# Attention and two feed-forwards on one core: another order of the last eight attention units, and an earlier load of the program's flag on VectorE

## The reference

```
scores = q @ k.T / 8 + alibi bias;  keep = key < 8 (global) or 0 <= query - key < 96 (local)
attention = softmax(where(keep, scores, -1e9)) @ v               # 8 heads of 64
h = x @ w_in;  g = (a0 + a1 h + a2 h^2 + a3 h^3) / (1 + |b0||h| + |b1| h^2 + 1e-6);  x = g @ w_out   # 512 -> 2048 -> 512
h = x @ w2_in; solu = h * softmax(h); out = layernorm(solu) * g_ln @ w2_out                           # 512 -> 1024 -> 512
```

## Time and profile before

| | us |
|---|---|
| median of 3 runs | 481.54 (480.85 to 481.79) |
| the profiled execution's own time | 480.79 |
| its span in the profile | 478.90 |
| TensorE busy in the span | 467.9 |
| VectorE busy in the span | 376.2 |
| ScalarE busy in the span | 270.0 |
| granted clock of TensorE, mean | 1.00 of full speed |

### The profile page before, as it was taken

The page is one execution under the profiler, slowest core; times in us unless marked ns, Lnnn a source line. Parts: engine busy times, 40 slices in busy tenths (PEclk is TensorE's granted clock), DMA queues, the critical chain, the costliest instruction groups (busy, mean ns, idle before and its releaser), DMA issues.

```text
span 478.9 us, 7527 instructions
## 1 busy us (share of the span) xinstructions
PE 467.9 (98%) x2734; PEld 382.6 (80%) x2734; DVE 376.2 (79%) x685; ACT 270.0 (56%) x477; POOL 60.4 (13%) x135
## 2 busy tenths in 40 slices
PE   7999989999999999999999999999999999999997
PEld 5667778888888878888887888888888888888885
DVE  6899989999999989778889999999685555555550
ACT  6999998656565555555556445443553333333341
POOL 5989850000000000000000000000000000000000
PEclk9999999999999999999999999999999999999999
DMA  8989864000000000000033445331012222222201
GB/s 294 365 323 335 297 239 179 1 0 1 0 1 0 1 1 0 1 1 1 5 105 89 139 138 170 104 88 44 10 35 67 66 66 66 74 67 76 68 23 44
DMA packets 25665, 42.91 MB, mean 90 GB/s; under 512 B 2080, under 2 KB 16800, under 8 KB 24480
## 3 DMA queue, kind: packets, MB, share of 16 engines
q1 hardware_dynamic: 23760, 36.64, 22.5%
q0 software_dynamic: 1296, 5.24, 3.6%
q10 hardware_dynamic: 576, 0.60, 0.4%
HBM read 33.04 MB, written 3.15 MB: 76 GB/s over the span
## 4 chain that ended last, share of the span: by engine, by line
PE 85%; ACT 8%; DVE 4%; issue 1%; DMA 0%; DVEq 0%; ACTq 0%
PE ps L1220 9%; PE ps L1221 9%; PE ps L1222 9%; PE ps L1152 8%; PE ps L1153 8%; PE ps L1154 8%; ACT probs L499 6%; PE ps L1285 5%; PE ps L1283 5%; PE ps L1284 5%; PE ps L1240 5%; PE ps L1239 5%; PE ps L1238 5%; PE ps L1266 2%; PE ps L1119 1%
## 5 line engine op out<-in xcount | busy, mean ns | idle before, releaser
L1220 PE MATMUL ps<-gate_hi,bank_b_hi 128*128 128x512 f32 x192 | 74.9, 390 | 0.5 <-DVE tok_lo L966 0.5
L1152 PE MATMUL ps<-tok_hi,bank_a_hi 128*128 128x512 f32 x192 | 75.0, 391 | 0.0
L1153 PE MATMUL ps<-tok_lo,bank_a_hi 128*128 128x512 f32 x192 | 74.7, 389 | 0.0
L1222 PE MATMUL ps<-gate_hi,bank_b_lo 128*128 128x512 f32 x192 | 74.7, 389 | 0.0
L1154 PE MATMUL ps<-tok_hi,bank_a_lo 128*128 128x512 f32 x192 | 74.7, 389 | 0.0
L1221 PE MATMUL ps<-gate_lo,bank_b_hi 128*128 128x512 f32 x192 | 74.7, 389 | 0.0
L562 ACT ACTIVATE quad<-ps 128x1024 f32<-128x1024 f32 x23 | 23.7, 1030 | 57.8 <-DVE rest L904 57.8
L499 ACT ACTIVATE probs<-negs,small 128x256 f32<-128x256 f32 (+1 forms) x96 | 45.9, 484 | 1.4 <-DVE small L743 1.1
L459 POOL TENSOR_SCALAR probs<-probs,small 128x256 f32<-128x256 f32 (+1 forms) x96 | 42.6, 467 | 10.7 <-DVE small L754 10.5
L886 DVE SCALAR_TENSOR_TENSOR quad<-quad,small,absh 128x1024 f32<-128x1024 f32 x23 | 29.5, 1282 | 17.9 <-ACT absh L565 17.8
L1220 PEld LDWEIGHTS ps<-gate_hi,bank_b_hi 128*128 128x128 f32 x192 | 36.0, 188 | 8.7 <-issue 1.2
(11 more groups left out here) (107 smaller groups left out, 945.5 us busy)
## 6 DMA issues: line engine op xcount, KB each, us to landing
v_sb<-in_v_win SPq DMA_DIRECT2D x8, 704.0 KB, 6.1
bank_a_raw<-in_w_in SPq DMA_DIRECT2D x4, 1024.0 KB, 8.7
bank_b_raw<-in_w_out SPq DMA_DIRECT2D x4, 1024.0 KB, 7.7
stage_hi<-tok_hi SPq DMA_DIRECT2D x12, 256.0 KB, 2.7
stage_lo<-tok_lo SPq DMA_DIRECT2D x12, 256.0 KB, 2.8
out_dram<-out_sb SPq DMA_DIRECT2D x12, 256.0 KB, 2.0
q_sb<-in_q_t SPq DMA_DIRECT2D x14, 192.0 KB, 4.8
k_sb<-in_k_win SPq DMA_DIRECT2D x7, 384.0 KB, 7.2
```

Of the source, the lines that this page charges most:

```text
L1152: pe.matmul(banks(bank, 1), bank_a_hi[:, f, ws], x_hi, start=(k == 0), stop=False)
L1153: pe.matmul(banks(bank, 1), bank_a_hi[:, f, ws], x_lo, start=False, stop=False)
L1220: pe.matmul(banks(4 + k, 1), bank_b_hi[:, f, ws], g_hi, start=first, stop=False)
L1222: mm = pe.matmul(banks(4 + k, 1), bank_b_lo[:, f, ws], g_hi, start=False, stop=last)
```

## The change

It has two parts.

1. **The tail.** ScalarE and VectorE leave their loops over pairs early and follow a written order, `attend_last`. TensorE takes the values of 40 to 43 at once after the transposition of 42 and 43, then `up(0)`, transposes 44 and 45, `up(1)`, transposes 46 and 47, takes the values of 44 to 47, then `up(2)`. `absh[1]` takes the place of `absh[0]` in the first group, since `absh[0]` lies over a buffer of probabilities. `TAIL` is 42. ScalarE's high parts there are of j = 2, 3, 4 and then 5, VectorE's low parts of tiles 4 to 6, 7 to 9, and 10 and 11.
2. **The head.** VectorE loads the flag before it waits for its two biases; the branch stays behind the two `attend_shift` of unit 0. The two `attend_shift` of unit 1 each wait for their own bias of the window and no longer both for the second.

```diff
 ScalarE
-            for n in range(0, HEADS, 2):
+            for n in range(0, TAIL - 2, 2):
                 attend_pair(n)
-            attend_out(HEADS - 4)
-            gate_first_inputs(0)
-            attend_out(HEADS - 1)
-            split_out_high(0)
-            gate_first_inputs(1)
+            attend_last()
+        def attend_last():
+            attend_copy(TAIL - 2)
+            for h in range(2):
+                attend_exp(HEADS - 2, h)
+            attend_out(TAIL - 4)
+            attend_copy(TAIL)
+            attend_out(TAIL - 1)
+            for h in range(2):
+                attend_exp(HEADS - 1, h)
+            for j in range(POOL_IN // 2, LATE_IN // 2 - 1):
+                split_in_high(j)
+            attend_copy(HEADS - 4)
+            gate_first_inputs(0)
+            split_in_high(LATE_IN // 2 - 1)
+            attend_copy(HEADS - 2)
+            attend_out(HEADS - 4)
+            gate_first_inputs(1)
+            attend_out(HEADS - 1)
+            split_out_high(0)
 VectorE
+        def attend_last():
+            attend_copy(TAIL)
+            attend_low(TAIL - 4)
+            attend_low(TAIL - 1)
+            attend_sums(HEADS - 2)
+            attend_reciprocals(HEADS - 2)
+            for f in range(POOL_IN, IDLE_IN - 2):
+                split_in_low(f)
+            attend_copy(HEADS - 4)
+            for f in range(IDLE_IN - 2, IDLE_IN + 1):
+                split_in_low(f)
+            attend_copy(HEADS - 2)
+            dve.wait_ge(coefs_loaded, 16)
+            dve.wait_ge(act_const, 1)
+            gate_first_poly(0)
+            attend_low(HEADS - 4)
+            attend_low(HEADS - 1)
+            gate_first_poly(1)
+            split_out_low(0)
+            for f in range(IDLE_IN + 1, LATE_IN):
+                split_in_low(f)
-            if h == 0 and n == 1:
-                dve.wait_ge(window_ready, 2)
+            if n == 1:
+                dve.wait_ge(window_ready, h + 1)
...
+        take = windowed(dve)
         dve.wait_ge(bias_ready, 2)
         for h in range(2):
             attend_shift(0, h)
-        take = windowed(dve)
...
-            for n in range(0, HEADS, 2):
+            for n in range(0, TAIL, 2):
                 attend_pair(n)
 TensorE
+            if n >= TAIL:
+                return
-            for n in range(0, HEADS, 2):
+            for n in range(0, TAIL + 2, 2):
                 attend_two(n)
-                if n == HEADS - 4:
-                    pe.wait_ge(shifted_ready, 2 * HEADS)
-                    up(0)
-            for n in (HEADS - 2, HEADS - 1):
+            for n in range(TAIL - 2, TAIL + 2):
                 attend_values(n)
             pe.wait_ge(shifted_ready, 2 * HEADS)
+            up(0)
+            attend_two(HEADS - 4)
             up(1)
+            attend_two(HEADS - 2)
+            for n in range(HEADS - 4, HEADS):
+                attend_values(n)
             up(2)
```

More of the change, by code:

```diff
@@ L250, in attention_feed_forwards @@
     LAG = 4
+    TAIL = HEADS - BLOCKS
     GROUPS = FT // 2
@@ L255, in attention_feed_forwards @@
     LATE_IN = FT - 4
-    IDLE_IN, END_IN = POOL_IN + 5, LATE_IN - 1
+    IDLE_IN = POOL_IN + 5
     def outs_at(n):
-        return [m for m in range(2, DONE_B0 - 1, 3) if n == m + (3 if m % 2 else 4)] + \
-            [m for m in (DONE_B0 - 1,) if n == HEADS - 4]
+        return [m for m in range(2, DONE_B0 - 3, 3) if n == m + (3 if m % 2 else 4)]
     HIGH_ON_DVE = (5, 14, 23, 32)
@@ L535, in attend_pair @@
                     attend_out(m)
-            if k < HEADS:
-                for h in range(2):
-                    attend_exp(k, h)
+            for h in range(2):
+                attend_exp(k, h)
             attend_copy(n)
-            if n == HEADS - 4:
[L541 to L545, removed]
+            for h in range(2):
+                attend_exp(k + 1, h)
+        def attend_last():
+            attend_copy(TAIL - 2)
+            for h in range(2):
+                attend_exp(HEADS - 2, h)
+            attend_out(TAIL - 4)
+            attend_copy(TAIL)
+            attend_out(TAIL - 1)
+            for h in range(2):
+                attend_exp(HEADS - 1, h)
[9 more added lines that the diff above has]
+            split_out_high(0)
         def gate_first_inputs(f):
@@ L551, in gate_first_inputs @@
             act.activation(quad[:, cs], src, ACT.Square).then_inc(first_in, 1)
-            act.activation(absh[0][:, cs], src, ACT.Abs, scale=coef_b[:, 0:1]).then_inc(first_in, 1)
+            act.activation(absh[1][:, cs], src, ACT.Abs, scale=coef_b[:, 0:1]).then_inc(first_in, 1)
             act.activation(poly[:, cs], src, ACT.Identity, scale=coef_a[:, 3:4],
@@ L793, in attend_pair @@
             pr, m = divmod(k, NPB)
[L794 to L801, removed]
-            attend_copy(n)
[L803 to L820, removed]
+            if pr and m == 0:
+                dve.wait_ge(pool_bias, 4 * pr - 2)
@@ new lines, in attend_pair @@
+            attend_shift(k, 0)
+            attend_shift(k, 1)
+            attend_copy(n)
+            attend_sums(n + SUMS_AHEAD)
+            if pr and m == 0:
+                dve.wait_ge(pool_bias, 4 * pr)
+            attend_shift(k + 1, 0)
+            attend_reciprocals(n + SUMS_AHEAD)
+            attend_shift(k + 1, 1)
+            for m_out in outs_at(n):
+                if m_out in HIGH_ON_DVE:
+                    attend_high(m_out)
+                attend_low(m_out)
+        def attend_last():
[19 more added lines that the diff above has]
+                split_in_low(f)
@@ L872, in gate_first_poly @@
             dve.wait_ge(first_in, 3 * f + 2)
-            dve.scalar_tensor_tensor(quad[:, cs], quad[:, cs], abs_b1, absh[0][:, cs], ALU.mult,
+            dve.scalar_tensor_tensor(quad[:, cs], quad[:, cs], abs_b1, absh[1][:, cs], ALU.mult,
                                      ALU.add).then_inc(quad_ready, 1)
```

## The result

The changed kernel is slower: 482.06 us (median of 16 runs, 481.79 to 483.48) against 480.99 for the kernel before, measured beside it (16 runs, 480.56 to 482.15). The ratio is 1.0024, with a 95% interval of 1.0015 to 1.0033, that is +1.15 us (+0.7 to +1.6). The profiled execution took 481.79 us, with a span of 480.0 against 478.9.

The account below looks back on a forecast made before the run. The kernel's end was taken to hang on VectorE's start of group 0's quotient, not TensorE's wait in attention. Tail +1.06 and head -0.18 gave +0.88 us, 482.4 from 481.54; range +0.48 to +1.44, 482.0 to 483.0.

Parts of the forecast that it names:

- slower: Whole-kernel outcome: slower than the kernel before by over 0.2%, 0.96 us; chance 0.38.
- within: Whole-kernel outcome: difference from the kernel before inside 0.2%, 0.96 us; chance 0.52.
- low 47: VectorE's low part of unit 47 in the tail: starts at 77.85 after waiting 0.23 for ScalarE's attend_out(47).
- quotient: VectorE's quotient of group 0, on whose start the kernel's end hangs: moves from 81.63 to 82.69, +1.06 us.
- gain of the head: Kernel start: the earlier flag load on VectorE gains 0.18 us; bounds 0.35 gained to 0.18 lost.
- TensorE's gain stands: Rival: the 0.67 us freed at the transposition of 42 carries to the end, -0.85 in all, 480.7; chance 0.14.
- terms of the tail: Steps on VectorE from the copy of 46 and 47 to group 0's quotient, making it +1.06 us later.
- 0.35 to win: Kernel start: the most gained if unit 1 needn't wait for VectorE's load, starting at 6.57 instead of 6.92.
- cover: VectorE's idle time just before group 0's quotient in the kernel before, waiting for ScalarE's exponential: 0.50 us.
- Nothing moves: Rival: head gives 0.35, VectorE does part of tiles 10 and 11 in time, quotient +0.5, about 481.7; chance 0.10.
- S: Start of VectorE's quotient of group 0: 81.63 before, forecast 82.69, +1.06 us.
- Later still: Rival: quotient later still, kernel measurably slower; a head giving nothing leaves +1.06, 482.6; decides from +0.96 on; chance 0.06.

Follow-up runs that it names:

- e3: Changed kernel with one extra VectorE subtraction of a 512-column tile between tile 11 and the first quotient; ratio to before 1.0042.
- e4: Kernel before with one extra VectorE subtraction of a 512-column tile between tile 11 and the first quotient; ratio to before 1.0002.
- e5: Changed kernel with VectorE's low parts of tiles 10 to 15 one group later, 10 and 11 behind group 0; ratio to before 0.9999.
- e2: Changed kernel with the head's change undone, so the tail alone; ratio to before 1.0041.
- e1: Kernel before with the head's change alone; ratio to before 1.0002.
- e10: Changed kernel, TensorE transposing 44 to 47 and taking their values between up(0) and up(1), other engines reordered, tiles 12 to 15 one group later; ratio to before 0.9976.
- e7: Kernel before with one move: ScalarE copies the pair 40, 41 before the exponentials of 46; ratio to before 0.9999.
- e9: Changed kernel with VectorE's tiles 10 and 11 behind group 2, 12 and 13 behind group 3, 14 and 15 behind group 4; ratio to before 0.9990.
- e6: Changed kernel with gate_first_poly(1) in front of the low part of unit 47 on VectorE; ratio to before 1.0013.

## Why the prediction was right

The forecast was +0.88 us within 0.48 to 1.44. Measured was +0.24%, +1.15 us, inside the range; the interval, +0.7 to +1.6, reaches a little beyond it. The trace gives +1.07 at `up(8)`. The mechanism was the one forecast, and the size was 0.2 us short. The measured value is just over the 0.2% that I had set as the bound of no change, so it falls into the case "slower", to which I had given 0.38, and not into the likeliest, "within", with 0.52; the interval holds the bound. The absolute forecast of 482.4 stood on a median of three runs, 481.54; the kernel before had 480.99 over 16 runs, and so the changed kernel came to 482.06 although the loss was larger than forecast.

| step | predicted, without the head's gain | measured, with it |
|---|---|---|
| transposition of 42 | 64.28 | 64.24 |
| up(0), held by low 41 | 67.19 | 67.26 |
| transposition of 46 | 73.74 | 73.74 |
| VectorE's copy of 46 | 74.51 | 74.50, after 1.10 of waiting |
| attend_out(44), attend_out(47) | 75.15, 77.25 | 75.15, 77.25 |
| low 47 | 77.85, waits 0.23 | 77.86, waits 0.16 |
| quotient | 82.69, +1.06 | 82.71, +1.08 |
| up(8) | +1.06 | 105.16, +1.07 |
| gain of the head | 0.18 | 0.07 at unit 1, 0.10 at unit 40 |

- **That the end hangs on the quotient** is shown by e3 and e4 (0.60 against 0.02 for the same tile) and by e5, where taking two tiles off the chain brings quotient and `up(8)` back. The rival that TensorE's gain stands is refuted with it. The waits of TensorE at `down(0)`, `up(6)` and `up(8)`, 1.17 against 0.12, are the same loss seen on the other engine.
- **The terms of the tail** added up to 1.06. The near match of the positions in the table flatters the forecast: with the head's 0.18 in it the quotient should have come at 82.5. Counted from the transposition of 40, which takes the head out, the quotient moved by 1.18 (e2: 1.25), so the tail was 0.12 short. It arose before `up(0)`: the transposition of 42 was 0.06 late by this count and `up(0)` 0.17, since it started 0.15 after low 41 ended (67.11), where I had 0.06. Of the 0.17, 0.07 came back up to the transposition of 46. The tail's 0.12 and the 0.08 by which the head fell short (0.10 at the transposition of 40, not 0.18) point the same way and make up the 0.2 that the forecast was short.
- **The other mis-sized term is the head.** I had unit 0's shift at 5.57 to 5.65; it started at 5.73, though the load was as long as read, 547 ns. What held it from 5.55 to 5.73 isn't settled: the trace names TensorE's scores, which end then, but in the kernel before the same shift started at 5.44 with scores that ended as late. So unit 0 was late by 0.29 and not by 0.17, and of the 0.35 to win 0.06 was left. e1 puts the head at under 0.1, e2 at up to 0.26. With 0.08 in place of 0.18 the forecast would have been +0.98, over the bound.
- **The cover** I had as 0.50; it was 0.6 (e4).
- **Rivals.** "Nothing moves" needed S at +0.5 and a head of 0.35; it had +1.08 and 0.1. "Later still" began, by the way I had put it, where the head's gain falls under 0.1. That is what the trace shows at the start of the kernel, and the tail was later than forecast besides, by 0.12. The mechanism of this rival is the forecast's own, VectorE's order behind the copy of 46 and 47, carried 0.1 further.

## What to carry to other kernels

Freeing the engine that the page shows as 98% busy gained nothing by itself here: ask which chain its next stage waits on, and count start to start what stands on that chain behind the moved wait. Small independent jobs, like splitting a weight tile, are the cover for such waits. When an order is changed they have to be dealt out again, so that they lie in the idle stretch (1.10 us was empty here) and not behind it. Where the other engines have been taken off the chain, as in e10, a better order on the busy engine does pay. To find out if a stretch has cover, put one more such job into it: 0.6 us at the end, or 0.02, is a clear answer where the change itself is at the edge of what can be measured.

## What the hardware showed that I had not expected

**Two starts.** The kernel before runs at about 480.7 or at about 481.9 us, and so do all variants in their own way (of the 16 runs of before beside the result 7 are over 481.5, of the changed kernel's 6 are over 482.9). The profiles of e4, e5, e7 and e9 fell in such a run and show where it arises, in the first 12 us. In e4 a transfer of keys for unit 2 landed late, and TensorE waited 1.56 us for it:

```profile
...
7.62 1.13 PE L1085 MATMUL ps<-k_sb,q_sb 64*128 64x256 f32 x8 [1.56 <-DMA k_sb<-in_k_win]
...
```

The granted clock of the stretches after it (third figure from the end) fell; from 6 to 8 us TensorE had been busy for 0.44 of 2.00:

```profile
...
8.00:10.00 2.00, 1.55 (x14) 1.08 (x12) 1.63 (x11) 1.16 (x5) 0.00 (x0) 0.95 1.05 427
10.00:14.00 4.00, 3.91 (x32) 2.98 (x30) 3.18 (x23) 3.65 (x16) 3.46 (x9) 0.60 1.01 406
14.00:20.00 6.00, 5.36 (x90) 4.16 (x90) 5.14 (x30) 6.00 (x24) 5.96 (x14) 1.00 0.83 275
...
```

Between 10 and 14 us its mean was 0.60, between the two levels of 2.4 and 1.2 GHz, and the transposition of 40 came at 63.76 and not at 62.37. In e7 TensorE waited 1.50 us for keys before its first scores, and the clock from 8 to 10 us was 0.50, the lower level; from 4 to 6 us TensorE had been busy for 0.50 of 2.00. The page "TensorE: Matmul & The Clock Gate" of the Trainium skill (section "What's actually happening") says that the clock takes one of these two levels by how busy the array has been. The two traces agree. In e5 and e9 eight matmuls of scores took 2.08 us instead of 1.14 while the clock's column says 1.00; that stays open. So does whether the late keys are the cause in e4, whose first eight matmuls of scores took 1.65 us already before the wait (1.24 in the kernel before). In e6 the same wait of 1.56 us came with an undisturbed clock, and no delay of that size followed. Both starts occur in every kernel, so they blur a difference of 0.2%, the more the fewer the runs, but don't make it: the ten early runs of the changed kernel lie at 481.79 to 482.19, the early ones of before at 480.56 to 481.02.

**The branch** on VectorE was short: 55 to 57 ns in the kernel before. The page "Advanced Engine Details and Errata" of the Trainium skill (section "Control Flow Timing") gives about 108 ns for a compare-and-branch; here the measurement decides. The load of the flag is the large part, 547 ns. ScalarE's load of 469 ns in the kernel before started at 5.0 and lay wholly beside its work on the bias, 0.91 us from 4.78. VectorE's in the changed kernel, also from 5.0, lay only in part beside its own biases, which end at 5.34.
